# One stage for linear attention and a dense layer: waves of 8 heads, dense matmuls between their merge steps, streamed dense weights

## What is computed

```python
def _attn_ref(q, k, v, beta) -> np.ndarray:
    k_n = k / (np.linalg.norm(k, axis=-1, keepdims=True) + 1e-06)
    ...
    for t in range(S):
        kt, vt, bt = (k_n[:, :, t], v[:, :, t], beta[:, :, t, None])
        y[:, :, t] = np.einsum('bhd,bhde->bhe', q[:, :, t], state)
        v_old = np.einsum('bhde,bhd->bhe', state, kt)
        state = state + bt[:, :, :, None] * np.einsum('bhd,bhe->bhde', kt, vt - v_old)
def _moe_ref(x, w_in, w_out) -> np.ndarray:
    h = x @ w_in
    sp = np.where(h > 20.0, h, np.log1p(np.exp(np.minimum(h, 20.0))))
    g = h * np.tanh(sp)
    return (g @ w_out).astype(np.float32)
def _moe2_ref(x, w_gate, w1, w2) -> np.ndarray:
    ...
    for e in range(E):
        h = np.maximum(x @ w1[e], 0.0)
        ye = h @ w2[e]
        out += P[:, e:e + 1] * ye
```

## Time and profile before

| | |
|---|---|
| median of 3 runs | 2579.06 us (2573.7 to 2584.87) |
| span of the profiled execution | 2573.7 us (its time is that of the fastest run shown) |
| PE busy | 2501.1 us, 97% |
| DVE, ACT, POOL busy | 1185.0, 873.6, 429.8 us |
| first merge product / first gate product of the experts | 20.21 / 939.54 us |
| mean granted clock of PE | 0.972 of full |

### The profile page before, as it was taken

How to read it: one execution, slowest core, us unless ns; L and a number is a source line. 1 busy time by engine, 2 the same in 40 slices (tenths; PEclk the granted TensorE clock), 3 DMA queues, 4 the chain that set the end, 5 groups by cost and what they waited for, 6 DMA issues and landing times.

```text
span 2573.7 us, 42037 instructions
## 1 busy us (share of the span) xinstructions
PE 2501.1 (97%) x16476; PEld 2233.1 (87%) x16476; DVE 1185.0 (46%) x2237; ACT 873.6 (34%) x1898; POOL 429.8 (17%) x350
## 2 busy tenths in 40 slices
PE   6989889989999989999999999999999999999999
PEld 5888888878888869899999998999999998999998
DVE  5766557678777744443333333333333333333332
ACT  5857557756666631111111111111111111111111
POOL 7665547300000011000000000000000000000100
PEclk8989779989999989999999999999999999999999
DMA  1110101020000000000000000000000000000001
GB/s 65 38 44 22 43 23 37 2 86 13 0 0 0 0 25 25 25 1 25 25 1 25 25 1 26 11 15 26 1 25 26 1 25 26 1 25 25 1 13 62
DMA packets 13737, 55.26 MB, mean 21 GB/s; under 512 B 1408, under 2 KB 4608, under 8 KB 11648
## 3 DMA queue, kind: packets, MB, share of 16 engines
q10 hardware_dynamic: 6624, 37.10, 4.1%
q1 hardware_dynamic: 6944, 15.58, 1.9%
HBM read 47.95 MB, written 4.72 MB: 20 GB/s over the span
## 4 chain that ended last, share of the span: by engine, by line
PE 61%; issue 2%; DVE 0%; POOL 0%; DMA 0%; ACT 0%; SPq 0%; POOLq 0%; DVEq 0%
PE ex_y L51 30%; PE ex_h L51 30%; PE ex_logits L51 0%; DMA ex_fold<-fold 0%; POOL ex_w_lo L903 0%; POOL ex_col L917 0%; DVE ex_col L989 0%; DVE ex_r_lo L1038 0%; DVE ex_prob L986 0%; DVE ex_prob L998 0%; DVE ex_row L980 0%; DVE ex_row L984 0%; DVE ex_col L996 0%; DVE ex_acc L1019 0%; ACT ex_r_hi L952 0%
## 5 line engine op out<-in xcount | busy, mean ns | idle before, releaser
L952 ACT ACTIVATE ex_r_hi<-ex_h 128x512 fp32r<-128x512 f32 x384 | 229.0, 597 | 1250.0 <-PE ex_h L51 1250.0
L1038 DVE SCALAR_TENSOR_TENSOR ex_r_lo<-ex_h,ex_r_hi 128x512 fp32r<-128x512 f32 x384 | 265.4, 691 | 760.3 <-ACT ex_r_hi L952 759.7
L51 PE MATMUL ex_y<-ex_w_hi,ex_r_hi 128*128 128x384 f32 x1536 | 517.3, 337 | 0.9 <-DVE ex_r_lo L1038 0.9
L51 PE MATMUL ex_y<-ex_w_hi,ex_r_lo 128*128 128x384 f32 x1536 | 518.2, 337 | 0.0
L51 PE MATMUL ex_y<-ex_w_lo,ex_r_hi 128*128 128x384 f32 x1536 | 515.9, 336 | 0.0
L51 PE MATMUL ex_h<-x_hi,ex_w_lo 128*128 128x512 f32 x1152 | 456.3, 396 | 0.0
L51 PE MATMUL ex_h<-x_lo,ex_w_hi 128*128 128x512 f32 x1152 | 455.4, 395 | 0.0
L51 PE MATMUL ex_h<-x_hi,ex_w_hi 128*128 128x512 f32 x1152 | 449.1, 390 | 0.7 <-issue 0.4
L903 POOL TENSOR_TENSOR ex_w_lo<-ex_stage,ex_w_hi 128x512 fp32r<-128x512 f32 x96 | 123.7, 1290 | 1759.0 <-ACT ex_w_hi L937 1723.6
L1019 DVE SCALAR_TENSOR_TENSOR ex_acc<-ex_y,ex_prob,ex_acc 128x384 f32<-128x384 f32 x340 | 210.0, 618 | 279.8 <-PE ex_y L51 279.7
L51 PEld LDWEIGHTS ex_y<-ex_w_hi,ex_r_hi 128*128 128x128 f32 x1536 | 288.6, 188 | 18.8 <-DVE ex_r_lo L1038 1.4
(11 more groups left out here) (124 smaller groups left out, 3220.5 us busy)
## 6 DMA issues: line engine op xcount, KB each, us to landing
ex_stage<-w_exp ACTq DMA_DIRECT2D x15, 1536.0 KB, 6.3
at_qT<-q_t ACTq DMA_DIRECT2D x10, 512.0 KB, 4.1
out<-ex_acc SPq DMA_DIRECT2D x6, 768.0 KB, 3.5
at_v_in<-v ACTq DMA_DIRECT2D x11, 384.0 KB, 3.0
at_k_in<-k ACTq DMA_DIRECT2D x10, 384.0 KB, 4.8
de_stage<-w_in SPq DMA_DIRECT2D x8, 384.0 KB, 3.3
de_stage<-w_out SPq DMA_DIRECT2D x8, 384.0 KB, 3.2
ex_stage<-w_exp SPq DMA_DIRECT2D x2, 768.0 KB, 5.0
```

What stands on the lines that cost most here:

```text
L51: return nc.tensor.matmul(out, lhsT, rhs, start=start, stop=stop)
L952: nc.scalar.activation(r[tb % 2][0][:, j, :], h_bank[j][:], ACT.Relu).then_inc(hi_ready, 1)
L1038: nc.vector.scalar_tensor_tensor(out=r[tb % 2][1][:, j, :], in0=h_bank[j][:], scalar=0.0, in1=r[tb % 2][0][:, j, :].bitcast(F32), op0=ALU.max,
```

## The change

`attention_phase` and `dense_phase` become one `mixed_phase`. A wave is now 8 heads (one batch), in 2 groups, so there are 24 waves. The stage has 30 slots, written out without a hardware loop. Slot s holds the 21 merge steps of wave s. From slot 5 on, every one of 24 positions of a slot also holds a third of an `h` or `y` step of the dense layer, 3 products, of a chunk of tokens whose attention is finished: four pieces `f` to a slot. Slots 0 to 4 so hold attention alone, slots 5 to 23 both, slots 24 to 29 dense alone. There is one `h` bank and three `y` banks beside two `M` and two `O` banks. The dense weights are split during slots 0 to 3 (`split`), written to a DRAM tensor `w_split` and read back piece by piece for every chunk (768 KB per piece). The norms of k of all waves come in slots 0 to 2 (`norm`). The constant halves of the X tiles are written once, in a tile of their own per round. The low part of g moves from DVE to POOL, and the queue of ACT holds g_hi, Exp, Ln and Exp of a piece before the next piece's g_hi.

```diff
-def attention_schedule():
+def mixed_schedule():
+    merge = ["T2"] + [(kind, i) for i in range(len(MERGES)) for kind in "XTZ"] + ["res", "corr"]
+    dense = [(kind, k, m) for k in range(4) for kind in ("h", "y") for m in range(3)]
     other = {
...
+        0: [("B2", 0)],
+        2: [("B2", 1)],
+        3: [("B3", 0)],
+        4: [("S", 0)],
...
+    norms = [1, 4, 7, 10, 13, 16, 19]
+    splits = [5, 10, 15, 20]
+    for at in range(len(dense)):
+        if at < len(merge):
+            out.append(("M", merge[at]))
+        out.append(("D", dense[at]))
         out += [("O", x) for x in other.get(at, [])]
...
+    FIRST = B + 1
+    LAG = 2
+    WB = 4
...
+            for s in range(FIRST + C * 4 + 1):
...
         def _(sp):
+            def load_w(n):
+                i = n % WB
+                if n < WB:
+                    sp.wait_ge(w_stored[i], 16 * (FC // WB))
+                else:
+                    sp.wait_ge(down_done, n - WB + 1)
+                sp.dma_start(wbuf[i][:].bitcast(F32), w_split[n % FC]).then_inc(w_loaded[i], 16)
...
         def _(pool):
+            def dense(kind, n, m):
+                if kind == "h" and m == 1 and 0 <= n - 1 < ND:
...
+                    pool.wait_ge(hi_ready, j + 1)
+                    nc.gpsimd.tensor_tensor(g_lo[j % GR][:], hg[:, j % 2, :], g_hi[j % GR][:].bitcast(F32),
+                                            ALU.subtract).then_inc(lo_ready, 1)
...
         def _(act):
-            def unit_columns(g, i):
...
-                nc.scalar.copy(pair_half(i, True, X[g]), pair_half(i, True, four(ident_h[:])))
+            def split(f):
+                if f > 0:
...
+                    act.wait_ge(wlo_ready, f)
+                    act.dma_start(w_split[f - 1], wbuf[(f - 1) % WB][:].bitcast(F32)).then_inc(w_stored[(f - 1) % WB], 16)
+                    load_stage(f + 1)
...
+                nc.scalar.copy(wbuf[f % WB][:].rearrange("p (t i) c -> p i t c", i=2)[:, 0],
+                               stage[f % 2].rearrange("p (t c) -> p t c", t=2)).then_inc(whi_ready, 1)
...
+            def dense(kind, n, m):
+                if kind == "h" and m == 0 and 0 <= n - 1 < ND:
...
+                    act.wait_ge(g_ready, j + 1)
+                    nc.scalar.copy(g_hi[j % GR][:], hg[:, j % 2, :]).then_inc(hi_ready, 1)
+                if kind == "h" and m == MC - 1 and n < ND:
...
+                    act.wait_ge(h_done, n + 1)
+                    nc.scalar.activation(en[:, n % 2, :], h_bank[:], ACT.Exp).then_inc(e_ready, 1)
+                if kind == "y" and m == 1 and n < ND:
+                    act.wait_ge(hn_ready, n + 1)
+                    nc.scalar.activation(e, e, ACT.Ln, bias=two[:]).then_inc(log_ready, 1)
...
+                    nc.scalar.activation(e, e, ACT.Exp, scale=-1.0).then_inc(rec_ready, 1)
...
         def _(dve):
+            def norm(s):
+                dve.wait_ge(squared, s + 1)
+                nc.vector.tensor_reduce(of_wave(ksum, s), kq[s % 2][:], AX.X, ALU.add).then_inc(summed, 1)
...
+            def split(f):
...
+                dve.wait_ge(whi_ready, f + 1)
+                nc.vector.tensor_tensor(parts[:, 1], stage[f % 2].rearrange("p (t c) -> p t c", t=2),
+                                        parts[:, 0].bitcast(F32), ALU.subtract).then_inc(wlo_ready, 1)
...
+            def dense(kind, n, m):
+                if kind == "h" and m == 0 and 0 <= n - 1 < ND:
...
+                    dve.wait_ge(rec_ready, j + 1)
+                    nc.vector.tensor_tensor(hg[:, j % 2, :], hg[:, j % 2, :], en[:, j % 2, :], ALU.mult).then_inc(g_ready, 1)
+                if kind == "y" and m == 0 and n < ND:
...
+                    dve.wait_ge(e_ready, n + 1)
+                    nc.vector.tensor_scalar(e, e, CAP, None, ALU.min).then_inc(capped, 1)
...
+                    nc.vector.scalar_tensor_tensor(out=e, in0=e, scalar=2.0, in1=e, op0=ALU.add,
+                                                   op1=ALU.mult).then_inc(n_ready, 1)
...
+                    nc.vector.tensor_tensor(hg[:, n % 2, :], h_bank[:], e, ALU.mult).then_inc(hn_ready, 1)
...
         def _(pe):
+            def dense(kind, n, m):
+                if kind == "h" and n < ND:
...
+                    if m == 0:
+                        pe.wait_ge(w_loaded[i], 16 * (n // WB) + 16)
+                        if n > 0:
+                            pe.wait_ge(hn_ready, n)
```

More of the change, by code:

```diff
@@ L51, in mm, with three @@
     return nc.tensor.matmul(out, lhsT, rhs, start=start, stop=stop)
-def attention_schedule():
-    n = len(MERGES)
-    merge = ["T2"] + [(kind, i) for i in range(n) for kind in "XTZ"] + ["res", "corr"]
-    other = {
[L68 to L72, removed]
-        5: [("B3", 1)],
[L74 to L87, removed]
-    }
+def three(nc, out, lhs, rhs, start=True, stop=True):
+    mm(nc, out, lhs[0], rhs[0], start=start, stop=False)
+    mm(nc, out, lhs[0], rhs[1], start=False, stop=False)
+    return mm(nc, out, lhs[1], rhs[0], start=False, stop=stop)
@@ L156, in attention_phase @@
[L156 to L170, removed]
+        O_BANKS = {"B1": (0,), "B2": (1,), "B3": (0,), "B4": (1,), "B5": (1,), "F1": (0,), "F2": (0, 1)}
@@ L324, in _, with load_stage @@
+            slots(merge, other, dense, norm, lambda *a: None)
         @block.scalar
         def _(act):
-            def unit_columns(g, i):
-                nc.scalar.copy(pair_half(i, True, X[g]), pair_half(i, True, four(ident_h[:])))
-            def merge(step, c, w):
-                if step == "T2" and isinstance(c, int) and c == 0 and w == 0:
+            def load_stage(f):
+                if f < FC:
+                    for t, w in enumerate((w_in, w_out)):
+                        act.dma_start(stage[f % 2][:, t * CH:(t + 1) * CH],
+                                      w[:, f * CH:(f + 1) * CH]).then_inc(staged[f % 2], 16)
@@ L333, in merge, with root, norm @@
+            def root(first, last):
+                act.wait_ge(summed, last)
+                nc.scalar.activation(rnorm[:, H * first:H * last], ksum[:, H * first:H * last], ACT.Sqrt).then_inc(rooted, 1)
+            root(0, B)
+            def norm(s):
+                if s == NW - 1:
+                    root(B, NW)
+                    nc.scalar.preload_act_table_set("natural_log_exp_and_others")
+            def merge(step, s):
+                if step == "T2" and s == 0:
                     act.wait_ge(ident_ready, 1)
@@ L470, in _ @@
+            slots(merge, other, dense, norm, split)
         @block.tensor
@@ L812, in experts_phase @@
+            slots(merge, other, dense, lambda *a: None, lambda *a: None)
 def experts_phase(nc, w_gate, fold, w_exp, out, x_hi, x_lo, MC, N, E, F):
```

819 lines of the change are left out of this document (376 added, 443 removed).

## The result

The changed kernel takes 2776.18 us (median of 4 runs, 2771.56 to 2780.56) against 2578.47 (2573.7 to 2584.87) for the kernel before: a ratio of 1.0767, with a 95% interval of 1.0752 to 1.0783. It is slower, as forecast, but by more than twice the 91 us that I had summed, and above the range.

The account below looks back on a forecast made before the run. PE was taken to bound the dense stage and wait only about 5 us per attention wave. 21 + 172 + 712 + 120 + 6 = 1031 us to the gate against 939.5, 91 later, so 2670 us; range 2625 to 2710.

Parts of the forecast that it names:

- the split into three parts: New stage: slots 0 to 4 attention alone 172 us, 5 to 23 both 712, 24 to 29 dense alone 120.
- the walk through a mixed slot: Slots 5 to 23, queues followed position by position: 37.4 us each, 32.1 PE work and 5.3 waiting; taken as 37.5.
- The ramp: Slots 0 to 4, attention alone: unfilled links, splits and norms give 157 us, plus 15 for clock, 172; bounds 130 and 205.
- 3 us of clock: Slots 0 to 4: PE gaps of 3 to 4 us lower the clock, 15 us added, spread evenly over the slots.
- a split, sized at 2.1: Early slots: each of 16 weight splits delays ACT and DVE copies, about 2.1 us on the chain, 34 us in all.
- The norms, sized at 6.5 per slot: Slots 0 to 2: DVE waits for POOL's squares behind rest and RT, so copies come about 6.5 us later per slot.
- The tail: Slots 24 to 29, dense alone: 20 pieces take 112 us, the ending 8, then 6 to the experts' gate.
- the series of one piece: Dense-alone slots: all of a piece's activation stands between its Exp and the next, 5.6 us where PE needs 4.07.
- reading the weights back: Dense pieces: reloading 768 KB takes 5.0 us, would allow about 4.6 per piece, and hides, so costs nothing.
- the loop: Attention of the kernel before: the hardware loop's jump lengthens three waves by 17.7 us each; dropping it saves 53 us.
- The cold ramp with waits that pile up: Rival, chance 0.15: half clock makes slots 0 to 4 40 us each, mixed slots cost 39; 2733 us.
- Overlap: Rival, chance 0.13: mixed slots 33.5 us, ramp 130, total 2543; with the rest standing, it turns at 32.7 us a slot.

Follow-up runs that it names:

- e2: Changed kernel with POOL's g_lo, NT, Z2, rest and RT cut to a sixteenth of their columns after first uses: 2699.34 us, ratio 1.0471.
- e1: Changed kernel with the g_lo subtract moved from POOL back to DVE, at the same place of the slot: 2771.24 us, ratio 1.0749.
- e3: Changed kernel with only 4 of the 16 dense weight pieces split and stored, later loads reusing them: 2747.58 us, ratio 1.0658.
- e6: Changed kernel with ACT's g_hi moved behind the next piece's Exp and POOL's g_lo 4 positions later: 2787.64 us, ratio 1.0818.
- e9: Changed kernel with the activation rewritten using a Square on ACT, and g_hi behind the next Exp, g_lo later, from slot 24 on: 2731.44 us, ratio 1.0599.
- e4: Kernel before the change with only its hardware loop over attention chunks 1 to 4 written out: 2524.85 us, ratio 0.9794.

## Why the prediction was wrong

**The direction and the split into three parts** held. Each of them came out longer, most of all the mixed slots.

**The step that failed** is the walk through a mixed slot, where the prediction put it that "DVE's minimum, product and h times it run from 624.93 to 626.89, 2.0 us in one piece". These durations were read in a stretch in which POOL had no instruction at all (x0 in the third line of the earlier trace rows); I carried them to one in which POOL is busy 54 of 123 us. Beside POOL the triple's three operations have a mean of 2.56 us together (0.715 + 1.153 + 0.692), and hg*en is 0.26 longer: 0.95 us per piece by the durations of e2, 3.8 per slot, of which the slot felt 3.4 (41.5 to 38.1 in e2). That is 64 of the 76 us. It is POOL's attention work that does this in the mixed slots, and not the move of g_lo to POOL: with g_lo back on DVE (e1) they take 41.8.

**The walk had a second gap, and its near hit is partly luck.** The first product of a dense triple costs PE 0.08 to 0.09 us more than I counted, about 2.0 us per slot. The walk held nothing for it, and yet 37.4 is only 0.7 below the 38.1 of e2, so other terms of the walk must have been too long, if PE's 2.0 lie on the slot's path, which no run tested. They would cover the rest of the gap, 0.6 us a slot. What makes the first product longer is not shown: it is the same behind fp16 and fp32 products of the attention.

The Trainium skill ("SBUF — State Buffer", section "Who interferes with whom") says that DVE shares a port pair with GpSimd as an exclusive lock: a DVE operation with two SBUF inputs contends with a GpSimd operation that reads SBUF, one in a 2-port mode contends with GpSimd too, and one with at most one SBUF input outside these modes does not. The traces agree for the first and the last: 1153 against 688 ns for the same operation with one operand moved to PSUM, 692 and unchanged for h times e. The minimum was stretched with one SBUF input; by the rule it would be in a 2-port mode, which no view here names.

**The ramp: corr of slot 4 at 207 instead of 193.** The first merge product came at 23.99, not at 21: 3.0 of the 14 us. Slots 0 to 4 then took 38.6, 40.9, 38.6, 39.6 and 25.3 us, where the sum had 36, 39, 39, 33 and 25 with 3 us of clock in each. In slot 0 the second group's first product stood still for 3.47 us for POOL's Z2. Slot 3 is the one clearly mis-sized: e3 has 25.3 for it without splits at a clock of 0.98, where the walk had 22, and about 5 us go with the half clock, where I had 3. That slots 1, 2 and 4 came out near is partly luck. Slot 4 ran at full clock, so my 3 us of clock stood in for a bare slot that was 3.3 too short, and in slots 1 and 2 a split, sized at 2.1, is worth at most 2.1 and 1.7 us, with part of the clock in it. The norms, sized at 6.5 per slot, fit the 6.5 to 7.4 us by which slots 1 and 2 of e3 stand above its slot 3 (with a clock of 0.84 to 0.86 in that price). Their mechanism, squares that wait behind rest and RT, is not borne out: e2 shortened both and gained nothing in slot 2 (38.8 us at a clock of 0.66, against 38.6 at 0.73).

**The tail, 126 predicted, 145.7 measured.** The mean distance of Exps is 6.33 us, not 5.6, which makes 14.6 of the 19.7 us; the rest lies ahead of the first Exp (0.7) and behind the last (18.4 to the gate, where the sum had 14). Most of the 14.6 is POOL again, in an operation that I had at 0.42:

```profile
1055.32 1.29 POOL L423 TENSOR_TENSOR de_g_lo<-de_hg,de_g_hi 128x512 fp32r<-128x512 f32 x1 [5.35 <-ACT de_g_hi L493]
...
1055.71 1.18 DVE L630 TENSOR_SCALAR de_en<-de_en 128x512 f32<-128x512 f32 x1 [1.24 <-ACT de_en L501]
```

POOL's g_lo, freed by g_hi, starts just ahead of the next minimum, which ends 0.28 us after it. Here the move of g_lo, to which the sum gave no price, is the cause: with it shortened (e2) the distance is 5.71 and the tail 131.4, with it on DVE (e1) 5.83 and 133.8. So the series of one piece, undisturbed, was sized about right. Taking g_hi out of it is worth less than e6 and e9 gained (20 to 21 us), since the minimum became short in them too.

**What was counted at nothing and was nothing:** reading the weights back (768 KB landed in 4.3 us), the experts. **What was sized right:** the loop, 53 predicted, 52.4 by e4 (2577.28 for the kernel before, measured beside it, less 2524.85).

**The rivals.** None of them came true. The cold ramp with waits that pile up came nearest in time (2733) but named the wrong place: slots 1 to 3 were cold and near its 40 us, yet its mixed slots of 39 had no mechanism behind them. Overlap did not win even with POOL's load gone: 38.1 is far above the 32.7 at which it would, and with the 2.0 us for first products PE alone needs about 34.1, by estimate.

## What to carry to other kernels

A duration belongs to the stretch in which it was read: before carrying it to a new place, see which other engines work there, and for DVE whether POOL does and where the operands lie. In the dense activation here the operations with all operands in SBUF were stretched, the minimum with its single input among them, and those with one in PSUM were not. A change that moves an operation to another engine (g_lo) can be harmless in one stretch and cost 12 us in the next. Two kinds of work that each keep PE busy did not add up to a fuller PE here, since their copies share in-order queues; count the waits behind each long operation, with its stretched duration. And measure a change against the best form of the kernel before: here one line, the unrolled loop, was worth 2%, and it hid a fifth of what the rest of the change cost.

## What was not expected of the hardware

- A hardware loop's jump cost 16.5 to 17.7 us a time in a 73 us body (three such waves, 52.4 us in all by e4). In the wave looked at PE stood still for 5.9 us of it, in two waits on "issue"; the rest goes with the lower clock, 0.72 over the wave.
- With the two engines colliding both pay. In e6 DVE's L632 rose to 1379 ns and POOL's g_lo to 1558, from 1153 and 1281.
- A 512-column dense product behind a shorter attention product took 0.31 us to the next start in place of 0.23, at 347 of 354 places in the mixed slots.
- Slot 4 came at either clock (0.99 to 1.00, or 0.72 over the slot) in kernels that are alike up to it, and was 25.3 or about 30 us long accordingly. What decides between them there stays open.
